# Writing out a hardware loop over block pairs in a fused attention and mixture-of-experts kernel

## The reference

```
phi(x)   = outer(S1 x, S2 x), flattened to 64 features      # S1, S2: 8 x 32
kv, z    = sum_s phi(k)^T v , sum_s phi(k)                  # per batch and head
attn     = (phi(q) kv) / (phi(q) z + 1e-6)                  # batch 4, heads 4, seq 1088, dim 32
x        = attn as 4352 tokens x 128
xn       = x / sqrt(mean(x^2) + 1e-6) * rms_g
y        = (silu(xn w_gate) * (xn w_val)) w_out             # 128 -> 1536 -> 128
logits   = y phi                                            # 32 slots
out      = softmax_over_slots(logits) @ experts(softmax_over_tokens(logits)^T y)
```

## Time and profile before

| | |
|---|---|
| median of 3 runs | 327.3 us (326.58 to 327.33) |
| profiled execution, its own time | 327.76 us |
| its span, first to last instruction | 326.0 us |
| what lies around the span | 1.76 us |
| PE busy | 304.7 us, 93% |
| DVE, ACT, POOL busy | 219.0, 176.3, 33.7 us |

### The profile page before, as it was taken

How to read it: one execution, slowest core, us unless ns; L and a number is a source line. 1 busy time by engine, 2 the same in 40 slices (tenths; PEclk the granted TensorE clock), 3 DMA queues, 4 the chain that set the end, 5 groups by cost and what they waited for, 6 DMA issues and landing times.

```text
span 326.0 us, 6844 instructions
## 1 busy us (share of the span) xinstructions
PE 304.7 (93%) x2596; PEld 245.7 (75%) x2596; DVE 219.0 (67%) x433; ACT 176.3 (54%) x333; POOL 33.7 (10%) x51
## 2 busy tenths in 40 slices
PE   1999599999999999999999999999999999997993
PEld 0788488877888888887878888888788778895572
DVE  4576766776676758767666777676677667874374
ACT  2559255556556565654655665566546655564410
POOL 1025491010010002001000100010010001001000
PEclk9999789999999999999999999999999999999998
DMA  6996048001000000099000000000000000000008
GB/s 181 301 330 178 4 179 336 1 2 64 0 2 1 3 0 2 4 284 287 4 0 0 0 0 0 0 0 0 0 0 1 0 2 0 3 0 3 2 29 247
DMA packets 25653, 19.97 MB, mean 61 GB/s; under 512 B 4128, under 2 KB 24352, under 8 KB 25632
## 3 DMA queue, kind: packets, MB, share of 16 engines
q1 hardware_dynamic: 25632, 19.68, 20.8%
HBM read 17.45 MB, written 2.23 MB: 60 GB/s over the span
## 4 chain that ended last, share of the span: by engine, by line
PE 84%; DVE 8%; DMA 2%; ACT 2%; issue 1%; SPq 1%; POOL 0%; DVEq 0%; ACTq 0%
PE bank L858 76%; PE bank L901 2%; DVE y_nat L849 2%; DMA area<-in_k 2%; PE bank L944 1%; DVE area L665 1%; PE bank L924 1%; PE bank L881 1%; DVE hl L700 1%; PE bank L1127 1%; DVE hid L694 1%; PE bank L1021 1%; SPq L309 0%; DVE area L759 0%; SPq L311 0%
## 5 line engine op out<-in xcount | busy, mean ns | idle before, releaser
L694 DVE TENSOR_TENSOR hid<-bank,silu 128x512 f32<-128x512 f32 (+1 forms) x108 | 71.5, 662 | 71.9 <-PE bank L858 57.7
L475 ACT ACTIVATE silu<-bank 128x512 f32<-128x512 f32 (+1 forms) x108 | 61.8, 572 | 74.4 <-PE bank L858 72.8
L700 DVE TENSOR_TENSOR hl<-hid,hh 128x512 fp32r<-128x512 f32 (+1 forms) x108 | 70.7, 655 | 0.1
L483 ACT ACTIVATE hh<-hid 128x512 fp32r<-128x512 f32 (+1 forms) x108 | 64.7, 599 | 0.8 <-DVE hid L694 0.8
L858 PE MATMUL bank<-xh,wgh 128*128 128x512 f32 (+1 forms) x117 | 47.1, 403 | 0.3 <-DVE xl L843 0.3
L858 PE MATMUL bank<-xh,wgl 128*128 128x512 f32 (+1 forms) x117 | 44.4, 380 | 0.0
L858 PE MATMUL bank<-xl,wgh 128*128 128x512 f32 (+1 forms) x117 | 44.2, 378 | 0.0
L858 PE MATMUL bank<-hh,woh 128*128 128x512 f32 (+1 forms) x108 | 43.8, 405 | 0.4 <-DVE hl L700 0.4
L858 PE MATMUL bank<-hh,wol 128*128 128x512 f32 (+1 forms) x108 | 41.1, 380 | 0.0
L858 PE MATMUL bank<-xh,wvl 128*128 128x512 f32 (+1 forms) x108 | 41.1, 380 | 0.0
L858 PE MATMUL bank<-xh,wvh 128*128 128x512 f32 (+1 forms) x108 | 41.1, 380 | 0.0
(11 more groups left out here) (150 smaller groups left out, 370.4 us busy)
## 6 DMA issues: line engine op xcount, KB each, us to landing
area<-in_moe_w SPq DMA_DIRECT2D x1, 4096.0 KB, 14.3
area<-in_moe_w SPq DMA_DIRECT2D x8, 512.0 KB, 7.3
area<-in_k SPq DMA_DIRECT2D x4, 512.0 KB, 6.3
y_nat<-in_v SPq DMA_DIRECT2D x4, 512.0 KB, 6.5
q_in<-in_q SPq DMA_DIRECT2D x4, 512.0 KB, 4.3
out<-y_nat SPq DMA_DIRECT2D x8, 256.0 KB, 2.9
area<-in_moe_w_gate SPq DMA_DIRECT2D x1, 768.0 KB, 8.6
area<-in_moe_w_val SPq DMA_DIRECT2D x1, 768.0 KB, 9.3
```

The costliest lines, as they stand in the source:

```text
L475: act.activation(silu[n][:, 0:w], gate_b[n][:, 0:w], ACT.Silu).then_inc(s_silu_ready, 1)
L483: act.activation(hh[m % NH][:, 0:w], hid[m % 2][:, 0:w], ACT.Copy).then_inc(s_hh_ready, 1)
L694: dve.tensor_tensor(hid[n][:, 0:w], val_b[n][:, 0:w], silu[n][:, 0:w], ALU.mult).then_inc(s_hid_ready, 1)
L700: dve.tensor_tensor(hl[m % NH][:, 0:w], hid[m % 2][:, 0:w], hh[m % NH][:, 0:w].bitcast(F32), ALU.subtract).then_inc(s_hl_ready, 1)
```

## The change

The three turns are written out on PE, DVE, ACT and GpSimd: `for b in range(1, B)` of Python in place of the hardware loop, so `b` is a number in every turn. With that go

- the register arithmetic in front of waits, and the compare-and-branch at the end of a turn;
- the tests that told a register from a number;
- the tile `kv_now`, its copy on GpSimd with the wait for `s_nd_ps` before it, and PE's wait for it. PE reads the moments from `kv[:, b, hp, :]`.

SyncE's stream keeps its loop. No compute instruction but the copy goes, none is added, and none changes its place in its engine's order. The tiles declared after `kv_now` (from `q_in` on) move down in on-chip memory by its 2 x 66 floats for each partition, 528 bytes before rounding.

```diff
-        kv_now = sb("kv_now", [P, HP, 2 * DA])
...
-        s_kvnow_ready = sem("kvnow_ready")
...
         def later(count):
-            return not isinstance(count, int) or count > 0
+            return count > 0
...
             inverse_rms(1)
-            with pool.Fori(1, B) as b:
-                pool.wait_ge(s_nd_ps, b * 2)
-                pool.tensor_copy(kv_now[:, :, :], kv[:, b, :, :]).then_inc(s_kvnow_ready, 1)
+            for b in range(1, B):
                 inverse_rms(b * 2)
                 combine_shift(b * 2 - 2)
                 inverse_rms(b * 2 + 1)
...
-            with act.Fori(1, B) as b:
+            for b in range(1, B):
                 whole_block(b * 2 - 1, 1)
...
-            with dve.Fori(1, B) as b:
+            for b in range(1, B):
                 whole_block(b * 2 - 1, 1, b)
...
             def attention(jn, b):
                 pe.wait_ge(s_qpT_ready, HP * jn + HP)
-                if not isinstance(b, int):
-                    pe.wait_ge(s_kvnow_ready, b)
...
-                            moments_of = kv[:, b if whole else 2 * t + x, hp, :] if isinstance(b, int) else kv_now[:, hp, :]
+                            moments_of = kv[:, b if whole else 2 * t + x, hp, :]
...
-            with pe.Fori(1, B) as b:
+            for b in range(1, B):
                 whole_block(b * 2 - 1, 1, b)
```

More of the change, by code:

```diff
@@ L288, in later @@
         def later(count):
-            return not isinstance(count, int) or count > 0
+            return count > 0
         def later_block(j):
-            return not isinstance(j, int) or j + 2 <= NB
+            return j + 2 <= NB
         def width(j):
-            return W if not isinstance(j, int) or j < NB else P * (NT - NB * HT)
+            return W if j < NB else P * (NT - NB * HT)
         block = ctx.enter_context(nc.Block())
@@ L471, in step @@
                 jm = j if m < C else j + 1
-                if m < C or not isinstance(j, int) or j < NB:
+                if m < C or j < NB:
                     w, n, i = width(jm), m % 2, C * j + m
@@ L477, in step @@
                 jm = j if m < C else j + 1
-                if m >= 0 and (m < C or not isinstance(j, int) or j < NB):
+                if m >= 0 and (m < C or j < NB):
                     w, i = width(jm), C * j + m
@@ L669, in split_x @@
                 w = width(jn)
-                if isinstance(jn, int) and jn == 0:
+                if jn == 0:
                     dve.wait_ge(s_small_loaded, 32)
@@ L720, in whole_block @@
                         logits(j - 1)
-                    if isinstance(j, int) and j == NB - 1 and c == 9:
+                    if j == NB - 1 and c == 9:
                         dve.tensor_reduce(cmax_a[:, :], logit[:, 0:NA, :].rearrange("p t s -> p s t"), axis=AX.X,
@@ L871, in queries_T @@
             def queries_T(jn, half, b):
-                if isinstance(jn, int) and jn == NB:
+                if jn == NB:
                     pe.wait_ge(s_qrem_loaded, 16 * B)
@@ L907, in attention @@
                 pe.wait_ge(s_qpT_ready, HP * jn + HP)
-                if not isinstance(b, int):
-                    pe.wait_ge(s_kvnow_ready, b)
                 for t in range(width(jn) // P):
                     for hp in range(HP):
-                        whole = not (isinstance(jn, int) and jn == NB)
+                        whole = not (jn == NB)
                         bk = (bank_a, bank_b)[t // 2] if whole else bank_a
@@ L957, in gate_value @@
                     pe.wait_ge(s_xl_ready, j + 1)
-                if isinstance(i, int) and i == 1:
+                if i == 1:
                     pe.wait_ge(s_kv_ready, B)
```

## The result

| | before | after |
|---|---|---|
| median of 7 runs | 327.08 us | 329.54 us |
| range | 326.26 to 328.0 | 328.11 to 330.22 |
| ratio | | 1.0070, 95% interval 1.0053 to 1.0087 |
| profiled execution | 327.76 us | 328.75 us |
| its span, and what lies around it | 326.0 and 1.76 | 326.6 and 2.15 |

A forecast was written before the change was run, and what follows sets the result against it. PE's matmul stream was taken to set the time from about 67 us. Profiled 327.76 us minus 0.09 for the copy, all other terms 0.0, gave 327.67; from the runs' median 327.3, 327.2 us; range 326.2 to 328.2.

The forecast's parts named there:

- Head and tail: Start and end of the kernel: same instructions in the same order, only tiles' places move; 0.0 us.
- Rival 2: Moved tiles change a DMA's or engine's rate, felt in the head: 325.2 or 329.2 us; chance 0.05 faster, 0.03 slower.
- Rival 3: Instruction loads fall behind data at 135.5 to 155 us, PE stands: 329.2 us, or 334; chance 0.03.
- The loop's own cost: PE's branches and wait arithmetic in the looped blocks, hidden under queued matmuls: 0.0 us gained, at most 4.2 us.
- rival 1: Register work or the jump back holds PE unseen: up to 4.2 us gained, more likely 325.1 us; chance 0.05.
- Instruction supply: PE's longer written-out program needs six or seven added instruction loads: 0.0 us, upper end 7 us.
- The copy beside DVE: Block 1's normalisation on DVE at 66.05 us, slowed by GpSimd's copy: 0.09 us gained, bounds 0 and 0.31.
- The prediction's other estimate: Block 1's normalisation on DVE, held by the shared port lock until the copy's end at 66.29: 0.24 us gained.

The follow-up runs named there:

- e2: Kernel before, loop and copy kept, with kv_now declared as the last tile: 329.68 us, ratio 1.0068 to the kernel before.
- e1: Changed kernel with an unused tile of kv_now's size where kv_now was: 327.26 us, ratio 0.9998 to the kernel before.
- k2: Changed kernel with 32-byte gaps ahead of wgh and ahead of q_in (weights at 0, moving operands at 64): 327.09 us, ratio 0.9995 to the kernel before.
- distance16: Changed kernel with a 32-byte gap after kv, and xh, xl, hh, hl widened by 16 floats and used from an offset: 29.75 to 29.84 us a block.
- low_weights_off: Changed kernel with a 32-byte gap after kv, and wgl, wvl, wol widened by 16 floats and used from an offset: 30.03 to 30.05 us a block.

## Why the prediction was wrong

**The step that failed** is "Head and tail. [...] Only tiles' places move. I take 0.0 us", and before it the tacit one that the same matmuls keep their pace. Rival 2 named the move of the tiles by 528 bytes (544 in the built program) and even the rate "of an engine", but priced its effect in the head alone, at 0.03 for slower; the effect is in the middle, 0.36 us for each whole block of 108 matmuls, 2.6 us in all. That the measured 329.5 us lies beside the 329.2 of rivals 2 and 3 is luck: the head and the instruction loads, which they priced, did not slow the kernel. I had the 0.23 us of a matmul in front of me and took it for a constant of the instruction. No row of the trace before could have shown the second value, since all of its matmuls of 512 columns lie at one distance.

**The loop's own cost**, 0.0 us: right. At equal places the written-out kernel has ratio 0.9998, and the looped one at the new places is as slow as the changed kernel (1.0068 against 1.0070). With that rival 1 fell. The Trainium skill's rule of loads after a taken branch (Runtime: NRT & Kernel Launch, section on instruction fetch) does not show here: e2 has 14 loads on q8, like the kernel before, and the loop costs nothing that can be measured. One reading in this part of the forecast was wrong and changes nothing: the 57 additions between 77.9 and 248.8 us come one in about 3.0 us, not 2.

**Instruction supply**, 0.0 us: right. q8 has 20 loads in place of 14; six fall in 137 to 246 us, and PE is full there. Rival 3 fell:

```profile
q8 instruction: 6, 0.10, 0.4%
```

```profile
137.00:155.00 18.00, 18.00 (x156) 14.32 (x155) 12.45 (x24) 9.10 (x17) 1.01 (x1) 1.00 1.05 263
```

**The copy beside DVE**, 0.09 us gained: right, within 0.02 us. In the chain the normalisation of block 1 takes 0.71 us in the two kernels with the copy and 0.62 in those without; here e2, then e1:

```profile
65.19 0.71 DVE area L665
```

```profile
66.15 0.62 DVE area L662
```

PE's wait for it must be compared at equal places: 0.47 us before against 0.40 in e1, 0.39 in e2 against 0.31 after, so 0.07 to 0.08 us of the 0.09 reached PE. The prediction's other estimate, 0.24 us, did not come.

**Head and tail, the rest**: two small terms that the forecast lacked, of opposite sign. In the looped kernels ACT stands 0.33 us ahead of `part_a` in the tail, in the written-out ones 0.05. Before, then e1:

```profile
298.37 0.33 issue
298.70 0.37 ACT part_a L564
```

```profile
298.08 0.05 issue
298.12 0.37 ACT part_a L561
```

That is 0.28 us gained. What it comes from, no run separates. And what lies around the span is 1.8 us in both looped kernels and 2.1 to 2.2 in the written-out ones, 0.35 us lost. Copy 0.09 and ACT 0.28 against 0.35 nearly cancel, which fits e1's ratio of 0.9998; sums this small can't be checked against an interval of 0.3 us either way.

## What to carry to other kernels

When an edit adds, drops or resizes a tile, compare the pace of identical matmuls (start to start) in the two traces before looking anywhere else: this kernel, bound by PE, lost 0.7% to where its operands start, with PE's busy time, share and clock all unchanged. To test an edit of code alone, keep the dropped tile as an unused one. Read the starts of all tiles out of the built program before you believe what a gap has moved: k2, distance16 and low_weights_off did not have the distances that they were meant to have. Here a hardware loop whose sequencer ran 2.75 us ahead of PE's matrix cost nothing, so writing it out had nothing to win.

## What the runs showed that I had not expected

A 128x128 by 512-column fp32r matmul took 229 ns where the moving operand starts 64 bytes above the weights' place (counted within 256 bytes) and 233 to 234 where it starts 32, 128, 160 or 192 bytes above it: a whole block 29.61 to 29.65 us against 29.97 to 30.06. It is the same with less than half of ACT's and DVE's work, and in code that is written out or looped. The times of single matmuls repeat in a short pattern, 226, 229, 232 ns in the fast kernels, and in the slow ones as 229 and 238 in turn (distance 128) or as 231 and 236 (distance 192). What in the hardware makes the pattern no run here shows.
